# First-layer products of a two-layer expert stage, issued in four sets of two instead of two sets of four

## What is computed

```python
for e in range(E):                       # 8 experts
    h = np.maximum(x @ w1[e], 0.0)       # x: 2304 x 512, w1[e]: 512 x 1024
    ye = h @ w2[e]                       # w2[e]: 1024 x 512
    out += P[:, e:e + 1] * ye
```

## Time and profile before

| | |
|---|---|
| median of 3 runs | 1045.05 us (1040.86 to 1045.7) |
| the profiled execution's own time | 1040.46 us |
| its span, first to last instruction | 1038.4 us |
| matmul busy | 1005.9 us, 97% of the span |
| weight loads busy | 926.5 us, 89% |
| VectorE busy | 755.6 us, 73% |
| GpSimd busy | 609.5 us, 59% |
| ScalarE busy | 583.1 us, 56% |
| last stage | from about 230 us to the end |

### The profile page before, as it was taken

The page is one execution under the profiler, slowest core; times in us unless marked ns, Lnnn a source line. Parts: engine busy times, 40 slices in busy tenths (PEclk is TensorE's granted clock), DMA queues, the critical chain, the costliest instruction groups (busy, mean ns, idle before and its releaser), DMA issues.

```text
span 1038.4 us, 25583 instructions
## 1 busy us (share of the span) xinstructions
PE 1005.9 (97%) x8667; PEld 926.5 (89%) x8667; DVE 755.6 (73%) x2042; ACT 583.1 (56%) x1368; POOL 609.5 (59%) x520
## 2 busy tenths in 40 slices
PE   8999988999989999999999999999999999999998
PEld 5787753469989999999989999999899999999998
DVE  6877742537898778777767788688668777878685
ACT  6677731244558656645664665465546564755552
POOL 5454530014586749666965697578647874977543
PEclk9999988989999999999999999999999999999999
DMA  5677248930200220022002200400130022000111
GB/s 186 228 269 285 73 163 339 408 143 2 82 2 1 83 82 2 2 83 83 2 4 86 79 2 2 156 8 1 52 116 1 2 81 84 2 2 22 62 41 62
DMA packets 36903, 87.79 MB, mean 85 GB/s; under 512 B 2976, under 2 KB 2976, under 8 KB 36768
## 3 DMA queue, kind: packets, MB, share of 16 engines
q1 hardware_dynamic: 36768, 86.07, 22.8%
HBM read 81.35 MB, written 4.72 MB: 83 GB/s over the span
## 4 chain that ended last, share of the span: by engine, by line
PE 60%; POOL 17%; issue 14%; DVE 5%; ACT 2%; DMA 1%; POOLq 0%; ACTq 0%; DVEq 0%
PE bank L783 13%; PE bank L785 12%; PE bank L787 12%; POOL s_split L491 11%; PE bank L733 4%; PE bank L560 3%; PE bank L570 3%; POOL t_split L496 3%; PE bank L589 3%; PE bank L670 2%; PE bank L607 1%; DMA mid_raw<-slot_w_in 1%; PE bank L677 1%; PE bank L711 1%; PE bank L601 1%
## 5 line engine op out<-in xcount | busy, mean ns | idle before, releaser
L491 POOL TENSOR_TENSOR s_split<-s_sum,s_split 128x512 fp32r<-128x512 f32 x288 | 372.1, 1309 | 322.2 <-ACT s_split L896 317.5
L1265 DVE SCALAR_TENSOR_TENSOR acc<-bank,gate_now,acc 128x256 f32<-128x256 f32 x441 | 227.1, 516 | 137.8 <-PE bank L787 136.5
L896 ACT ACTIVATE s_split<-s_sum 128x512 fp32r<-128x512 f32 x288 | 181.6, 632 | 248.5 <-PE bank L787 127.7
L783 PE MATMUL bank<-t_split,s_split 128*128 128x256 f32 x1008 | 283.4, 281 | 2.9 <-DVE acc L1265 1.7
L785 PE MATMUL bank<-t_split,s_split 128*128 128x256 f32 x1008 | 281.3, 279 | 0.0
L787 PE MATMUL bank<-t_split,s_split 128*128 128x256 f32 x1008 | 281.2, 279 | 0.0
L783 PEld LDWEIGHTS bank<-t_split,s_split 128*128 128x128 f32 x1008 | 191.3, 190 | 7.6 <-issue 5.7
L787 PEld LDWEIGHTS bank<-t_split,s_split 128*128 128x128 f32 x1008 | 189.5, 188 | 0.0
L785 PEld LDWEIGHTS bank<-t_split,s_split 128*128 128x128 f32 x1008 | 189.3, 188 | 0.0
L783 PE MATMUL bank<-t_split,a 128*128 128x256 f32 x576 | 162.1, 281 | 5.3 <-DVE acc L1259 2.7
L785 PE MATMUL bank<-t_split,a 128*128 128x256 f32 x576 | 160.5, 279 | 0.0
(11 more groups left out here) (171 smaller groups left out, 1973.7 us busy)
## 6 DMA issues: line engine op xcount, KB each, us to landing
raw<-big_w_in SPq DMA_DIRECT2D x15, 2048.0 KB, 8.7
slot_raw<-slot_w_in SPq DMA_DIRECT2D x14, 1024.0 KB, 6.7
mid_raw<-slot_w_in SPq DMA_DIRECT2D x6, 1024.0 KB, 10.1
early_raw<-slot_w_in SPq DMA_DIRECT2D x6, 1024.0 KB, 11.0
late_raw<-slot_w_in SPq DMA_DIRECT2D x6, 1024.0 KB, 8.3
q_ring<-q_tiles SPq DMA_DIRECT2D x18, 256.0 KB, 5.1
k_ring<-k_tiles SPq DMA_DIRECT2D x18, 256.0 KB, 5.3
v_ring<-v_rows SPq DMA_DIRECT2D x18, 256.0 KB, 2.7
```

The source lines that it names most:

```text
L491: pool.tensor_tensor(s_split[:, i, 1, :, :], s_sum[:, i, :, :], s_split[:, i, 0, :, :].bitcast(F32), ALU.subtract)\
L783: pe.matmul(to, left[:, 0, f, :], t_place(parity, k, 0)[:, f, :], start=(f == 0 and k in FRESH), stop=False, skip_group_check=k not in FRESH)
L896: act.activation(s_split[:, i, 0, :, :], s_sum[:, i, :, :], ACT.Copy).then_inc(s_hi_ready, 1)
L1265: done = dve.scalar_tensor_tensor(out=to, in0=got, scalar=gate, in1=to, op0=ALU.mult, op1=ALU.add)
```

## The change

`hidden` gets an argument that picks one of its two halves (two matmuls into one bank). TensorE calls it ahead of products 0, 1, 2 and 3, one half each. VectorE's `sums_first` stands behind additions 1 and 3 instead of 0 and 2, and `sums_second` behind 2 and 4 instead of 1 and 3. ScalarE, GpSimd and SyncE are as before. Line numbers shift by one.

```diff
-            def hidden(e, p, parity, s, n, before):
+            def hidden(e, p, parity, s, n, before, halves=(0, 1)):
-                for b, f, quarter in ((4 + 2 * s, HF + 2 * s, 2 * s), (3 + 2 * s, 2 * s, 2 * s + 1)):
+                sets = ((4 + 2 * s, HF + 2 * s, 2 * s), (3 + 2 * s, 2 * s, 2 * s + 1))
+                for b, f, quarter in [sets[i] for i in halves]:
...
-                        if ahead and k == 0:
-                            hidden(e1, p1, parity1, 0, n1, before)
-                        if ahead and k == 2:
-                            hidden(e1, p1, parity1, 1, n1, before)
+                        if ahead and k < 4:
+                            hidden(e1, p1, parity1, k // 2, n1, before, halves=(k % 2,))
...
                         add_product(e, p, k, parity, first)
-                        if ahead and k in (0, 2):
+                        if ahead and k in (1, 3):
                             sums_first(n1, (parity1 + p1) % 2, k // 2, before)
-                        if ahead and k in (1, 3):
-                            sums_second(n1, (parity1 + p1) % 2, k // 2, before)
+                        if ahead and k in (2, 4):
+                            sums_second(n1, (parity1 + p1) % 2, k // 2 - 1, before)
```

## The result

| | before | changed |
|---|---|---|
| median, us (runs) | 1042.05 (8) | 1049.04 (8) |
| lowest to highest | 1040.4 to 1045.7 | 1046.33 to 1051.14 |
| profiled execution, us (span) | 1040.46 (1038.4) | 1050.02 (1047.9) |
| mean granted clock | 0.988 | 0.983 |

The ratio is 1.0062, 95% interval 1.0045 to 1.0079: slower by 0.6%, 7.0 us between the medians where 6.1 were forecast. In a second session (experiment 10) it was 1.0054 (1.0038 to 1.0070).

The account below looks back on a forecast made before the run. TensorE was taken to set the end, matmuls covering 97% of the span. Terms 5.8 - 0.8 + 0 + 1.1 = +6.1 us, above a mean of 1043.0, gave 1049.1; range 1039.5 to 1055.

Parts of the forecast that it names:

- The chain at the end of an expert: Behind experts 0, 1, 3, 5, 6: L1178 starts 1.16 us later, A22 waits as much longer; +5.8 us.
- Rival D: At expert ends, A22 does not wait for the chain's start; total 1043, same, chance 0.08.
- The loop's two boundaries: Behind experts 2 and 4: addition 1 directly follows addition 0, so product 4 comes earlier; -0.8 us (0 to -1.2).
- the chain's shift is covered: At the loop's two boundaries, T4 is ready with over 3 us to spare, so the later chain adds no wait.
- Expert 0: Pairs with long gate rounds on VectorE: later sums delay A11, earlier additions compensate; 0 (-0.4 to +0.6 us).
- A11 then waits for L1167 behind them instead of addition 4: 0: In expert 0, behind gate rounds after product 4: A11 waits for the last sum instead, at no cost.
- The rhythm: TensorE's 113 and 118 ns start distances: shares unchanged, fast one entered twice a pair; +1.1 us (0 to 2.1).
- Each set of matmuls of another shape flips it, however short: On TensorE, every first-layer set between products switches the start distance, giving four flips a pair.
- Rival B: On TensorE, two matmuls do not flip the rhythm and it settles fast: -14, with waits -9, 1034; chance 0.13.
- the entries: On TensorE, each entry into the fast rhythm loses 0.03 us, now twice a pair instead of once; up to 2.1.
- A's premise: In pair 2, the fourth half set and `g_products` act as one flip: -4.8, total +1.3, 1044.3; chance 0.25.

Follow-up runs that it names:

- experiment 10: The changed kernel, unedited, run again beside the kernel before: 1047.57 us, ratio 1.0054.
- experiment 1: The changed kernel with VectorE's sums back at their old places, so TensorE's half sets alone: 1035.93 us, ratio 0.9951 to the kernel before.
- experiment 5: The changed kernel with GpSimd's T4 remainder of the next expert formed in pair 8, one pair earlier: 1042.94 us, ratio 1.0011 to the kernel before.
- experiment 11: The changed kernel with GpSimd's T4 remainder of pair 0 computed twice, only the second released to TensorE: 1066.78 us, ratio 1.0228 to the kernel before.
- experiment 3: The changed kernel with VectorE's old order of sums in expert 0 only: 1041.63 us, ratio 1.0011 to the kernel before.
- experiment 4: The changed kernel with each half set issued twice, four matmuls into one bank: 1109.08 us in one execution.
- experiment 2: The kernel before, sets of four kept, with only VectorE's sums one product later: 1053.34 us, ratio 1.0117.
- experiment 7: The changed kernel with each half set issued three times, six matmuls into one bank: 1159.32 us in one execution.
- experiment 8: The changed kernel with each half set's second matmul issued twice, three into one bank: 1076.48 us in one execution.

## Why the prediction was right, and where it was not

- **The chain at the end of an expert**: right. Forecast +1.16 at each of five boundaries; measured 1.26 on average at A22 of experts 2, 4, 6 and 7 (from 0.91 to 2.17 between starts). With the half sets alone this gap is 1.16 (experiment 1), so 1.01 of the 1.26 come with the later sums and 0.25 with TensorE's order. Experiments 5 and 11 show the cause: move T4's remainder and the wait at A22 goes, double it and the wait grows by 2.4. Rival D falls. Behind expert 0 the size was right (+1.0), but product 3 waits there, for VectorE's addition, and not A22 for T4.
- **The loop's two boundaries**: forecast -0.8, measured +0.7 in one execution and +2.9 in the other; in the first a stretch at 1.2 GHz lies ahead of product 3 of expert 3 and stands in the place of a wait (0.43 us, and 1.98 in the second). The step that failed is "the chain's shift is covered". For TensorE it was, but the later T4 now lies beside L1111 (L1110 in the changed kernel), which went from 1.68 and 1.26 to 2.7 to 3.0 us and holds up addition 0.
- **Expert 0**: forecast 0, at most +0.6; experiment 3 gives 3.95. The step that failed is the last one there, "A11 then waits for L1167 behind them instead of addition 4: 0". The last sum stands not in the place of addition 4 but behind it, with two more sums: three steps of 0.33. A11 of pairs 3, 5 and 7 now waits 1.98, 2.94 and 1.57 us, where it waited under 0.3, 2.43 and 0.79; that makes some 3.2. Behind the rounds of product 2 (A11 of pairs 4 and 6) it waits 0.55 and 0.81, where 0.2 were forecast.
- **The rhythm**: forecast +1.1, measured -7.1 with the first layer's own distance. "Each set of matmuls of another shape flips it, however short" carried what sets of 4 and more do over to sets of 2. Those sets have no other shape, either: L733 is 128x256 as a product's matmuls are. Rival B's mechanism was the true one, at half its price (8 of 14 us): with the entries, a block of 12 takes 1.38 and not 12 x 0.1133 = 1.36, four times a pair, and expert 0 and the first pairs gain less. Next to a set of two `g_products` doesn't flip the rhythm any more either, so A's premise falls here; next to a set of four into one bank the two do act as one flip (experiment 4, expert 4: product 2 takes 1.42 us ahead of them, products 4 to 6 take 1.36 each behind).
- **The clock**: not in the sum; 6.2 us in the profiled execution, 1.5 in the second. No instruction that was moved costs it: longer waits bring it, in some executions and places and not in others.

Against 6.1 forecast the profiled accounts give 11.1: waits 12.0 for 5.0, clock 6.2 for 0, rhythm -7.1 for +1.1. Between the medians, where fewer stretches at 1.2 GHz weigh in, it is 7.0. Two costs left out and a gain forecast as a small loss cancelled; that 1049.1 and 1049.04 agree so closely is luck. So, in part, is the direction. Experiments 1 and 2 show that the later sums cost more than the rhythm gives. But the waits that the forecast counted, the boundaries' +6.0 and the loop's +0.7, are less than what the start distances give back (-7.1, and -8.2 with the short gaps): by themselves they would have left the kernel about where it was. It is slower by expert 0's waits (+5.2), forecast at 0, and by the clock (+6.2 and 1.5). Experiment 3, which takes back expert 0's part alone and whose profiled execution has no stretch, is at 1.0011 (0.9996 to 1.0027), not distinguishable from the kernel before.

## What to carry to other kernels

Take apart a change that touches two queues before judging it: here TensorE's new order alone gains 0.5 to 0.6%, and the matching delay on VectorE, which looks like slack in every steady pair, loses 1.2% where the queue behind it is full. Cost the boundaries and the first pass one by one, put every moved step behind all that is now ahead of it, and look for the engine that it will run beside. Where waits of the busiest engine grow to 2 us, take a term of some 1.5 us for the clock behind a part of them, and read more than one execution before ascribing it.

## What the runs showed of the hardware

- A stream of 128x256 products has two steady start distances here, 113 and 118 ns. Sets of four first-layer matmuls in between change from one to the other, whether into one bank or two; behind sets of two and three the fast one holds, and sets of six mostly left either as it was (experiments 1, 4, 7, 8). The Trainium skill ("TensorE: Matmul & The Clock Gate", Back-to-back issue gap) says that weight load and matmul set the distance together, and its formula for the isolated gap gives 109.2 ns; neither distance agrees with that figure, and what makes the two is open.
- TensorE's granted clock stood at 1.2 GHz for mostly 16 matmuls behind some of the waits of 2.0 us and more, and behind all four above 4 us (experiment 11); 16 of them cost 1.55 us.
- VectorE's weight remainder, which reads two operands of SBUF, waits for the whole GpSimd instruction under way: it ended 1.08 or 1.09 us behind that one's end in 98 of 98 cases, and took 2.79 us where GpSimd's had just begun (experiment 10) and 1.68 where that had nearly ended.
